# Scores of the first three levels as 32-key by 16-query halves on eight tiles of the TensorE array

## Time and profile before

| what | value |
|---|---|
| median of 3 runs | 956.94 us (955.68 to 957.22) |
| the profiled execution | 958.38 us |
| its span, first to last instruction | 956.4 us |
| mean granted TensorE clock | 0.982 of full speed |
| TensorE matmuls | 911.5 us busy, 10824 instructions |
| VectorE / ScalarE / GpSimd busy | 530.8 / 398.5 / 148.0 us |

### The profile page before, as it was taken

One profiled execution on the slowest core, in us unless ns is written; L12 is line 12 of the kernel. 1 busy time (PEld: TensorE's weight loads), 2 busy tenths in 40 slices (PEclk: granted clock), 3 DMA queues, 4 the chain that ended last, 5 costly groups with the idle time before them and its releaser, 6 DMA issues.

```text
span 956.4 us, 24664 instructions
## 1 busy us (share of the span) xinstructions
PE 911.5 (95%) x10824; PEld 882.3 (92%) x10824; DVE 530.8 (56%) x993; ACT 398.5 (42%) x805; POOL 148.0 (15%) x151
## 2 busy tenths in 40 slices
PE   0679799999999999999999999999999999999998
PEld 0669699999999999999999999999999999999998
DVE  6655688866867767767767764464222222222322
ACT  1322365555544644645544544574222232222222
POOL 2320503403403404305205100000000000000000
PEclk9968899999999999999999999999999999999999
DMA  9940570160160260250430200512011011010000
GB/s 270 234 111 27 173 110 3 26 127 2 27 126 2 51 102 2 64 89 2 84 69 2 51 3 1 207 42 75 1 50 50 1 50 50 1 51 25 1 25 25
DMA packets 112554, 57.69 MB, mean 60 GB/s; under 512 B 92480, under 2 KB 108096, under 8 KB 111936
## 3 DMA queue, kind: packets, MB, share of 16 engines
q1 hardware_dynamic: 112448, 56.11, 24.5%
HBM read 45.09 MB, written 11.01 MB: 59 GB/s over the span
## 4 chain that ended last, share of the span: by engine, by line
PE 92%; DVE 5%; DMA 1%; ACT 1%; issue 1%; SPq 0%; DVEq 0%; ACTq 0%
PE bank L1075 17%; PE bank L1077 15%; PE bank L1076 15%; PE bank L1312 10%; PE bank L1311 10%; PE bank L1310 10%; PE bank L1013 5%; PE bank L1024 2%; PE bank L1050 2%; PE bank L1056 1%; PE bank L1037 1%; PE bank L982 1%; PE bank L987 1%; DMA first_q<-in_q_dram 1%; PE bank L992 1%; PE bank L1070 1%
## 5 line engine op out<-in xcount | busy, mean ns | idle before, releaser
L1280 DVE TENSOR_TENSOR product<-bank,a_copy 128x384 f32<-128x384 f32 x64 | 35.7, 557 | 219.1 <-PE bank L1312 219.1
L1075 PE MATMUL bank<-x_hi,w_in_hi 128*128 128x384 f32 x384 | 135.5, 353 | 0.5 <-DVE x_lo L896 0.5
L1075 PE MATMUL bank<-g_hi,w_out_hi 128*128 128x384 f32 x384 | 133.6, 348 | 0.3 <-DVE g_lo L907 0.3
L1077 PE MATMUL bank<-x_hi,w_in_lo 128*128 128x384 f32 x384 | 129.3, 337 | 0.0
L1076 PE MATMUL bank<-x_lo,w_in_hi 128*128 128x384 f32 x384 | 129.2, 336 | 0.0
L1077 PE MATMUL bank<-g_hi,w_out_lo 128*128 128x384 f32 x384 | 128.7, 335 | 0.0
L1076 PE MATMUL bank<-g_lo,w_out_hi 128*128 128x384 f32 x384 | 128.6, 335 | 0.0
L1312 PE MATMUL bank<-y_hi,w_lo 128*128 128x384 f32 x384 | 128.3, 334 | 0.0
L1310 PE MATMUL bank<-y_hi,w_hi 128*128 128x384 f32 x384 | 128.3, 334 | 0.0
L1311 PE MATMUL bank<-y_lo,w_hi 128*128 128x384 f32 x384 | 128.3, 334 | 0.0
L653 ACT ACTIVATE g_hi<-gated 128x384 fp32r<-128x384 f32 x128 | 67.2, 525 | 128.1 <-DVE gated L902 128.0
(11 more groups left out here) (113 smaller groups left out, 1759.9 us busy)
## 6 DMA issues: line engine op xcount, KB each, us to landing
v_leaf<-in_v_dram SPq DMA_DIRECT2D x8, 576.0 KB, 6.5
v_rows<-in_v_dram SPq DMA_DIRECT2D x64, 72.0 KB, 2.8
middle<-middle_out SPq DMA_DIRECT2D x8, 576.0 KB, 2.8
w_rows<-in_moe_w_dram SPq DMA_DIRECT2D x8, 512.0 KB, 10.4
f_leaf<-in_f_logit_dram SPq DMA_DIRECT2D x28, 144.0 KB, 3.9
k_leaf<-in_k_dram SPq DMA_DIRECT2D x28, 144.0 KB, 4.7
q_leaf<-in_q_dram SPq DMA_DIRECT2D x28, 144.0 KB, 4.2
out_dram<-out_rows SPq DMA_DIRECT2D x7, 576.0 KB, 3.3
```

The source lines that it names most:

```text
L1075: nc.tensor.matmul(o, w[0], b[0], start=first, stop=False)
L1077: return nc.tensor.matmul(o, w[1], b[0], start=False, stop=last_)
L1280: nc.vector.tensor_tensor(pf[:, f % RING], b_bank[f % 2][:, 0:UNIT], af[:, f % 2], ALU.mult)\
```

## The change

At levels 0, 1 and 2 each call is replaced by two: keys 0 to 31 of the chunk with the 16 later-half queries of tokens 0 to 31, and keys 32 to 63 with the 16 of tokens 32 to 63. They land on PSUM partitions `to` to `to + 31` in columns `o` to `o + 15`, and on `to + 32` to `to + 63` in columns `o + 16` to `o + 31`; that is where the same scores stood before. The other two quarters of each 64 x 32 block are no longer written. The first halves of the four heads of `corners` are issued first, then the four second halves, so that eight different 64-row by 32-column tiles of the array are used in turn. Level 3 issues what it did. VectorE clears both banks once at the start, since the predicated copy still reads the whole of them, and TensorE waits for that before its loop. Nothing else changes: the same steps at the same positions.

```diff
--- before.py
+++ after.py
@@ -17,6 +17,7 @@
 
 
 
+import itertools
 from contextlib import ExitStack
 
 import concourse.bass as bass
@@ -196,6 +197,7 @@
         constants = ctx.enter_context(nc.semaphore("constants"))
         pool_chain = ctx.enter_context(nc.semaphore("pool_chain"))
         mask_sum = ctx.enter_context(nc.semaphore("mask_sum"))
+        banks_clear = ctx.enter_context(nc.semaphore("banks_clear"))
         w_landed = [ctx.enter_context(nc.semaphore(f"w_landed{i}")) for i in range(KD + WO_LOADS)]
         w_last_in, wl_hi, wl_lo, turned, turned_hi, turned_lo, joined, joined_ev, y_first_in = (
             ctx.enter_context(nc.semaphore(n)) for n in (
@@ -733,6 +735,7 @@
         def _(dve):
             nc.vector.memset(state[:], 0.0).then_inc(middle_free, 1)
             nc.vector.memset(scores[:], 0.0).then_inc(mask_sum, 1)
+            nc.vector.memset(wide[:, :, 0:CHUNKS * PAIRS // 2 * HALF], 0.0).then_inc(banks_clear, 1)
             dve.wait_ge(middle_free, 1)
             dve.wait_ge(mask_sum, 1)
 
@@ -1003,16 +1006,19 @@
                         wait(pe, "k_next", u, n)
                     for m in range(CHUNKS):
                         at_ = m * CHUNK
-                        for i in range(PAIRS // 2):
+                        for i, of in itertools.product(range(PAIRS // 2), range(2 if n < LEVELS - 1 else 1)):
                             for ab, pair in corners(i):
                                 o = (pair % 2 * CHUNKS + m) * HALF
-                                later_half = qd[head_rows(ab), pair, at_:at_ + CHUNK]\
+                                if n < LEVELS - 1:
+                                    part, cols, tokens_ = of, HALF // 2, slice(at_ + of * HALF, at_ + (of + 1) * HALF)
+                                else:
+                                    part, cols, tokens_ = 0, HALF, slice(at_, at_ + CHUNK)
+                                later_half = qd[head_rows(ab), pair, tokens_]\
                                     .rearrange("p (b h c) -> p b h c", h=2, c=c)[:, :, 1]
-                                keys = HALF if n == LEVELS - 1 else CHUNK
-                                to = score_half(ab, pair).start
-                                last = nc.tensor.matmul(wide[to:to + keys, pair // 2, o:o + HALF],
-                                                        kw[head_rows(ab), pair, at_:at_ + keys], later_half,
-                                                        start=True, stop=True)
+                                to = score_half(ab, pair).start + part * HALF
+                                last = nc.tensor.matmul(wide[to:to + HALF, pair // 2, o + part * cols:o + (part + 1) * cols],
+                                                        kw[head_rows(ab), pair, at_ + part * HALF:at_ + (part + 1) * HALF],
+                                                        later_half, start=True, stop=True)
                     last.then_inc(sems["level_mm"], 1)
                 elif kind == "krow":
                     wait(pe, "k_next", u, LEVELS)
@@ -1140,6 +1146,7 @@
                     up(1, u)
 
             pe.wait_ge(constants, CONSTANTS)
+            pe.wait_ge(banks_clear, 1)
             for pos in range(FIRST, ROUND * UNITS):
                 u, h = pos // ROUND, pos % ROUND
                 if pos >= 0 and h == 0:
```

## The result

The changed kernel took 1042.92 us (median of 4 runs, 1039.73 to 1046.85) against 957.08 us of the kernel before (4 runs, 955.68 to 957.77). The ratio is 1.0903, 95% interval 1.0874 to 1.0931. The forecast was 962.0 us: slower it is, but by 86 us where 5 had been worked out. The profiled execution took 1039.73 us, its span was 1037.8 us, 81.4 us more than before.

What follows compares the result with a forecast made beforehand. The prediction took TensorE, busy 95% of the span, to bound the kernel. Its 4.6 us (units 1 to 7) and 0.44 us (unit 0) made 5.1 us on the median of 956.94: 962.0 us, range 958.9 to 964.3.

Steps and rivals of the forecast that it cites:

- More instructions: Instruction supply for 4608 added loads and matmuls: taken as zero, at most a share of 1.07 us a changed level.
- Instructions run short: Rival: changed levels outrun instruction supply, half a packet's time each, 13 us in all, 975 us; chance 0.04.
- The levels' pace: Changed levels at full clock: 1.76 us against 1.54, +0.22 us each, +4.6 us over 21 in units 1 to 7.
- The prediction's bound from above: Pace of a changed level: 8.4 ns from the first matmul on, 1.61 + 0.15 = 1.76 us.
- eight at once, but the issue rate holds: Rival: first 32 matmuls at 6.7 ns, 160 at 8.4, 1.67 us a level, 959.0 us; chance 0.18 with another mild case.
- main case: Changed levels: added matmuls run at the late 8.4 ns pace, eight tiles bring no gain; around 962.0 us, chance 0.70.
- The rule of about 60 cycles an instruction: Skill page's cost per matmul: doubling the count would add some 30 us; the prediction held its size disagreed with the trace.
- Unit 0: First and third level counted in full, +0.44 us; second level, at half clock, 2.59 against 2.56 us, nothing.
- The clearing: VectorE's memset of the banks at the start: about 0.7 us, hidden in idle time before GpSimd's masks, cost nothing.
- The fourth level: Level already with 32-key weights, not changed: expected to stay at 0.95 us.

Runs made afterwards that it cites:

- same_count_64_keys: Changed kernel with its 192 matmuls a level kept, but each with all 64 keys as weights on four 64x64 tiles; 1048.93 us, ratio 1.0966.
- fourth_level_twice: Kernel before with the fourth level's calls issued twice (192 matmuls on four tiles), first three levels untouched; 979.6 us, ratio 1.0241.
- filled_to_boundaries: Changed kernel plus 434 small calls on one tile, placed so levels of units 1 to 7 pass one block boundary each; 1025.96 us, ratio 1.074.
- filled_rotating_tiles: Changed kernel plus 434 small calls between the steps of units 1 to 7, going round four tiles in turn; 1012.34 us, ratio 1.0613.
- Shifted_half_block: Changed kernel with 32 small calls (128 instructions) before TensorE's loop, moving all block boundaries by half a block; 1018.1 us, ratio 1.0641.

## Why the prediction was wrong

**The stall, and its double price.** The step that failed is "More instructions". It saw that the 0.95 us of the 32-key level show the supply only over 192 instructions, "not over twice that", and then took zero "by the 32-key level, the nearest row", with a share of one packet's 1.07 us a level as the bound from above. Both were wrong: 47.8 us of waiting is 2 us a changed level, twice that bound. A packet's own duration doesn't bound a wait for it. In unit 1's first level the first boundary (29 matmuls) is passed at 131.55, no packet is under way until 134.2, it has ended by 135.7, and TensorE goes on at 137.12: the packet itself takes 1.5 of those 5.6 us (5.8% of 16 engines over 1.6 us), 2.7 pass before it and 1.4 behind it. The rival "Instructions run short" named the mechanism, but with half a packet a level, 975 us, and a chance of 0.04. The rows for another reading were there: 86 packets for 21,648 loads and matmuls are one for every 252, or about 256 with the waits that the view doesn't count, more than an old level's 192 and less than a new one's 384. No place of the trace of before used 256 matmuls and loads in less than about 4.4 us, counted start by start, so the zero was an extrapolation, and the page of the Trainium skill quoted above names the block and would have turned the row into a rival of size.

**The clock** was in no step: most stops of 2 to 5 us are followed by half clock. The mean granted clock gives its length, (1 - 0.949) x 2 x 1037.8 = 106 us at half clock in after, (1 - 0.982) x 2 x 956.4 = 34 us in before. The difference costs at most half its length, 36 us (at most, since part of that time is the waiting itself). The traces show where it lies: from 127 to 650 us the kernel before has no half clock, and in after there are 14 stretches of it, 72 us in all, each beginning in a stop or within 2 us behind one. The same three terms, read from each run's own waits, timeline and clock, account for each run to within 7 us:

| kernel | span over before's 956.4 | "issue" | longer levels, calls | half clock, at most | sum |
|---|---|---|---|---|---|
| after | 81.4 | 47.8 | 4.5 | 36 | 88 |
| same_count_64_keys | 92.1 | 28.4 | 33.3 | 34 | 96 |
| fourth_level_twice | 22.5 | 9.4 | 6.4 | 6 | 22 |
| filled_to_boundaries | 63.6 | 15.4 | 40.7 | 11 | 67 |
| filled_rotating_tiles | 49.7 | 23.5 | 20.8 | 8 | 52 |

(Third column: 23 levels by 1.73 - 1.53, or 24 by 2.92 - 1.53 us with 64 keys; 8 by 0.80; 36.2 and 16.3 us for the small calls.) Shifted_half_block has 36.6 + 4.5 + 22 = 63 for 58.8, with 8 us less waiting for w_rows in unit 0.

**The levels' pace** was right. A clean level takes 1.73 us, forecast 1.76, or +0.20 us for +0.22. (The prediction's bound from above, 8.4 ns from the first matmul on, took 0.15 us behind the last one where its other sums take 0.12; with 0.12 it is 1.73, what was measured.) Its inner course is that of the second rival, "eight at once, but the issue rate holds". Windows of line 1019 in the clean level of unit 1, as in the earlier trace rows:

```profile
157.29:157.46 0.17, 0.16 (x31) 1.00 0.00 0
157.29:158.00 0.71, 0.70 (x85) 1.00 0.00 0
157.29:158.92 1.63, 1.62 (x192) 1.00 0.00 0
```

31 matmuls start in 0.17 us, 5.5 ns each, against 7.9 on four tiles: eight tiles do run beside each other, as "TensorEngine Tiling (Array Packing)" of the Trainium skill has it under Tiling Modes, where its eight 64x32 tiles are listed too (not in the Overview that the prediction names). From the 85th on, 107 take 0.92 us, 8.6 ns; start by start most steps are 16.7 ns for two, 8.33 ns, with a few longer ones. So the main case's cause (only four loads in flight) was wrong and its number held by the issue pace, which is the same for 16 and 32 moving columns and for four and eight tiles. Above it no tile order helps: 192 x 8.33 ns = 1.60 us is already more than the 1.39 us that 96 of the 64-key shape take. That is why even without a stop the change costs 4.5 us, and no version of it was found that would beat the kernel before. The rule of about 60 cycles an instruction ("Instruction Overhead" on the same page) remains far too large for these small matmuls on tiles in turn, as the prediction held; on one and the same tile they start 32 ns apart (filled_to_boundaries). Sixty cycles at 2.4 GHz would be 25 ns, an estimate from that page's figure, so there the rule is not too large.

**Unit 0.** The first and the third level take 1.73 us, as forecast. The second, forecast at no change, has two of the stops (0.5 and 5.3 us). Timeline of TensorE in after, answering to the earlier trace rows:

```profile
47.00 0.64 PE L1019 MATMUL bank<-q_cols,k_cols 48*32 48x16 f32 x55 [3.19 <-DVE scores L859]
48.12 1.43 PE L1019 MATMUL bank<-q_cols,k_cols 48*32 48x16 f32 x128 [0.48 <-issue]
54.87 0.31 PE L1019 MATMUL bank<-q_cols,k_cols 48*32 48x16 f32 x9 [5.32 <-issue]
```

**The clearing** was right: hidden, at 3.70 us for 0.70 us, and measured alone as nothing. The fourth level was right as well.

## What to carry to other kernels

Count instructions, not only columns: before a dense stretch of small matmuls is lengthened, compare its number of loads and matmuls with the 256 of a block, and the time in which it uses a block with the 3 to 5.6 us that the next one took here. Several short stretches with long products between them were free here where one long stretch was not, and a few instructions added far away move all the boundaries: this kernel lost or won 25 us by 128 of them. And where a term is priced at zero because the trace shows none of it, ask how far outside the observed range the new case lies; a stop of some microseconds costs TensorE's clock besides.

## What the runs showed that was not expected

- On eight tiles small matmuls start 5.3 to 5.5 ns apart for the first 32 and 8.33 ns apart afterwards; on four tiles it is 7.9 ns and then the same late pace (8.4 ns in the earlier trace rows). The Trainium skill, "Advanced Engine Details and Errata", Engine Queue Depths, gives TensorE a queue of 64, which is 32 pairs; the change of pace in the trace lies there.
- On one single tile small fp32 matmuls of 32 weight columns start 32 ns apart, four times as far as on four tiles in turn (filled_to_boundaries: 36 of them in 1.31 us; filled_rotating_tiles: 0.49 us, less 0.2 for the last one in both).
- The clock falls after some stops, not after all: in after the one of 1.7 us in unit 7's first level is followed by it, the one of 2.4 us in unit 4's second level is not. What decides between them was not settled.
- A block takes 2.9 us in one place and 5.6 in another, and what differs most is how late its packet starts after the boundary before. In the first levels of units 1 to 6 of after it is 1.2 to 2.7 us, and the queue of the inputs moves 0.26 to 0.43 MB between the boundary and the packet; in the second levels, where that queue moves at most 0.06 MB in between, it is 0.8 to 1.1 us. Unit 7's first level, with no inputs left to load, has 0.5 us and the shortest of the stops in first levels (timeline of TensorE; then the DMA queues from 614.8 to 617.8 us). That the input loads hold the packet back fits this and was not tried by a run of its own.

```profile
614.88 1.26 PE L1019 MATMUL bank<-q_cols,k_cols 48*32 48x16 f32 x128
617.83 0.82 PE L1019 MATMUL bank<-q_cols,k_cols 48*32 48x16 f32 x64 [1.69 <-issue]
```

```profile
q8 instruction: 1, 0.02, 1.9%
```
